# Two banks of 288 columns for each head's scores, and turned tails in the free columns of the PV banks

## The reference, cut to what matters

```python
# q, k, v: (4 batches, 8 heads, 576 tokens, 64)
scores = q @ k.T / 8
thresh = max(scores) - tau
scores = where(scores >= thresh, scores, -1e9)
attn = exp(scores - max(scores)); attn /= sum(attn) + 1e-9
x = attn @ v                        # per head, then (4, 576, 512)
u = x + (relu(x.T @ w_tok1) @ w_tok2).T      # mixing over tokens
y = u + relu(u @ w_ch1) @ w_ch2
h = relu(y @ w_in); z = h * sigmoid(conv3(h)); out = z @ w_out
```

## Time and profile before

| | |
|---|---|
| median of 3 runs | 868.86 us (868.48 to 869.29) |
| profiled execution | 868.8 us, span of the core 867.0 us |
| granted TensorE clock, mean | 0.996 |
| TensorE matmul busy | 826.0 us, 95% of the span, 5512 instructions |
| VectorE, ScalarE, GpSimd busy | 420.9, 411.0, 263.7 us |
| chain that ended last | PE 86%, DVE 5%, ACT 4%, issue 4% |

### The profile page before, as it was taken

The page is one execution under the profiler, slowest core; times in us unless marked ns, Lnnn a source line. Parts: engine busy times, 40 slices in busy tenths (PEclk is TensorE's granted clock), DMA queues, the critical chain, the costliest instruction groups (busy, mean ns, idle before and its releaser), DMA issues.

```text
span 867.0 us, 14725 instructions
## 1 busy us (share of the span) xinstructions
PE 826.0 (95%) x5512; PEld 655.8 (76%) x5512; DVE 420.9 (49%) x829; ACT 411.0 (47%) x866; POOL 263.7 (30%) x202
## 2 busy tenths in 40 slices
PE   7889899999999999799999999999999999999998
PEld 3556566666666666678888888888899989898996
DVE  6787777777777773621121121121122908246280
ACT  4787777777778775311111111121112737356471
POOL 0063323232232321472020020030092645528180
PEclk9999999999999999899999999999999999999999
DMA  9311111111111114000000000000230010010101
GB/s 267 112 50 50 50 51 48 48 48 48 48 48 48 48 17 147 1 1 0 1 1 1 0 1 1 1 0 1 110 85 2 2 50 1 25 36 0 48 0 60
DMA packets 20906, 33.75 MB, mean 39 GB/s; under 512 B 4416, under 2 KB 11136, under 8 KB 20864
## 3 DMA queue, kind: packets, MB, share of 16 engines
q1 hardware_dynamic: 20864, 33.18, 11.8%
HBM read 28.46 MB, written 4.72 MB: 38 GB/s over the span
## 4 chain that ended last, share of the span: by engine, by line
PE 86%; DVE 5%; ACT 4%; issue 4%; DMA 1%; POOL 0%; DVEq 0%; ACTq 0%; SPq 0%; POOLq 0%
PE score L1142 17%; PE score L1253 12%; PE score L987 5%; PE out_t L1157 4%; PE turn_y L1157 4%; PE mixed L1157 4%; PE tails L1157 4%; PE out_t L1053 4%; PE out_t L1238 4%; PE mixed L1053 4%; PE mixed L1099 3%; PE score L1010 3%; PE turn_y L1238 3%; PE mixed L1238 3%; PE tails L1238 3%
## 5 line engine op out<-in xcount | busy, mean ns | idle before, releaser
L903 DVE SCALAR_TENSOR_TENSOR h<-score,h 128x512 fp32r<-128x512 f32 (+1 forms) x60 | 38.3, 638 | 246.6 <-ACT h L683 246.6
L683 ACT ACTIVATE h<-score 128x512 fp32r<-128x512 f32 (+1 forms) x60 | 33.3, 555 | 256.5 <-PE score L1142 256.5
L824 DVE TENSOR_SCALAR_CACHE_REDUCE negs<-score,neg_scale 128x576 f32<-128x576 f32 x144 | 112.6, 815 | 73.5 <-PE score L987 44.8
L841 DVE SCALAR_TENSOR_TENSOR prob<-negs,thresh,exps 128x576 f32<-128x576 f32 x144 | 133.7, 960 | 0.3 <-ACT thresh L595 0.3
L592 ACT ACTIVATE exps<-negs,neg_max 128x576 f32<-128x576 f32 x144 | 104.7, 772 | 2.2 <-DVE negs L824 1.5
L1142 PE MATMUL score<-uh,w1h 128*128 128x512 f32 (+1 forms) x240 | 89.2, 372 | 6.1 <-DVE ul L873 6.1
L1142 PE MATMUL score<-ul,w1h 128*128 128x512 f32 (+1 forms) x240 | 89.0, 371 | 0.0
L1142 PE MATMUL score<-uh,w1l 128*128 128x512 f32 (+1 forms) x240 | 89.0, 371 | 0.0
L560 POOL TENSOR_TENSOR zl<-z,zh 128x512 fp32r<-128x512 f32 x32 | 54.8, 1712 | 98.1 <-ACT zh_t L762 98.1
L1010 PEld LDWEIGHTS score<-ident,prob 64*128 64x128 f32 x512 | 41.0, 139 | 45.3 <-issue 45.2
L987 PE MATMUL score<-qk 64*128 64x512 f32 x256 | 72.3, 641 | 0.0
(11 more groups left out here) (179 smaller groups left out, 2001.0 us busy)
## 6 DMA issues: line engine op xcount, KB each, us to landing
qk<-in_qk SPq DMA_DIRECT2D x16, 704.0 KB, 4.1
vm<-in_v SPq DMA_DIRECT2D x16, 320.0 KB, 4.4
result<-ostage SPq DMA_DIRECT2D x16, 256.0 KB, 2.1
w1f<-in_moe_w_ch SPq DMA_DIRECT2D x4, 768.0 KB, 11.0
w2f<-in_moe_w_ch SPq DMA_DIRECT2D x4, 768.0 KB, 8.1
wif<-in_moe_w_in SPq DMA_DIRECT2D x1, 2048.0 KB, 7.9
wof<-in_moe_w_out SPq DMA_DIRECT2D x8, 256.0 KB, 2.6
wt2f<-in_moe_w_tok SPq DMA_DIRECT2D x1, 576.0 KB, 9.8
```

The source lines that it names most:

```text
L824: nc.vector.tensor_scalar(negs[:, i, h, :], raw_of[h], neg_scale[:, 0:1], None, ALU.mult, ALU.min, accum_out=neg_max[:, i, h:h + 1]).then_ ...
L841: nc.vector.scalar_tensor_tensor(out=prob[:, i, h * S:(h + 1) * S], in0=negs[:, i, h, :], scalar=thresh[:, i, h:h + 1], in1=exps[i][:, h, ...
```

## The change

The scores of a head take two banks, 288 columns in each, with products of 64 rows in four parts (column half c, head h). The product for the tails goes, and with it the doubled k in the input, in which the second head's keys are laid so that its last 64 come first. The waits on `max_done` come one per head. Bank 3 of `score` now belongs to the scores, and the bank once called `tails` (now `turn_x`) takes one half of the turned probabilities. The turned tails go to columns 288 and up of `out_t` and `mixed`: tile 0's in two turns of 64 rows ahead of the PV products, tile 1's behind them, tiles 2 and 3 in s = 2 and 3. ScalarE drains them in four copies where there was one. The output turned back goes to `out_t` in one bank, and the second half of `mix_out(1)`, which is computed in the order mixed, out_t, waits until that is drained.

```diff
-        turn = [score[:, 3, :], turn_y[:, :]]
-        raw = score[:, 0:3, :].rearrange("p b c -> p (b c)")
-        raw_of = [raw[:, 0:S], raw[:, 2 * BANK - TAIL:3 * BANK]]
+        turn = [turn_x[:, :], turn_y[:, :]]
+        raw_of = [score[:, 0:2, 0:HALF], score[:, 2:4, 0:HALF]]
...
-            def drain_tails(at):
-                act.wait_ge(tail_turned, FULL * (at.g + 1))
-                nc.scalar.activation(probTt[at.par][:, 0:MAIN], tails[:, :], ACT.Copy).then_inc(tails_drained, 1)
+            def drain_first_tails(at):
+                if at.k == 0:
+                    act.wait_ge(tail_turned, 2)
+                nc.scalar.activation(probTt[at.par][:, 0:D], mixed[:, TAIL_AT:TAIL_AT + D], ACT.Copy).then_inc(tails_drained, 1)
+                nc.scalar.activation(probTt[at.par][:, D:2 * P], out_t[:, TAIL_AT:TAIL_AT + P + D], ACT.Copy) \
+                    .then_inc(tails_drained, 1)
+            def drain_tail(at, t):
+                act.wait_ge(tail_turned, FULL * at.g + t + 1)
+                bank = out_t if t == 2 else mixed
+                nc.scalar.activation(probTt[at.par][:, t * P:(t + 1) * P], bank[:, TAIL_AT:TAIL_AT + P], ACT.Copy) \
+                    .then_inc(tails_drained, 1)
             def drain_out(pair, k):
                 act.wait_ge(pv_done, pair + 1)
+                if k < PAIRS - 1:
+                    act.wait_ge(tail_turned, FULL * (pair + 1) + 2)
...
-                nc.scalar.activation(uy_pair[:, pair, 0:MAIN], tails[:, :], ACT.Copy).then_inc(xt_drained, 1)
+                nc.scalar.activation(uy_pair[:, pair, 0:MAIN], out_t[:, :], ACT.Copy).then_inc(xt_drained, 1)
...
-            def score_tails(unit):
...
-                    nc.tensor.matmul(raw_tails, qT[par][:, t * P:(t + 1) * P],
-                                     kd[par][:, :].rearrange("p (n c) -> p n c", c=TAIL))
...
+            def scores(unit):
...
+                    for c in range(2):
+                        for h in range(2):
+                            if t >= 1 and c == 0:
+                                pe.wait_ge(max_done, tiles_to(g, t) - 1 + h)
+                            rows = slice(h * D, (h + 1) * D)
+                            mm = nc.tensor.matmul(score[:, 2 * h + c, 0:HALF], qT[par][rows, t * P:(t + 1) * P],
+                                                  kT[par][rows, halves[c]])
                 else:
+                    pe.wait_ge(max_done, tiles_to(g, t) - 1)
+                    for c in range(2):
+                        mm = nc.tensor.matmul(score[:, c, 0:HALF], qd[par][:, :], kT[par][:, halves[c]])
...
+            def turn_first_tails(at):
+                wait_for_banks(at)
+                pe.nop(nofuse=True)
+                for r, bank in enumerate((mixed, out_t)):
+                    rows = slice(r * D, (r + 1) * D)
+                    mm = nc.tensor.transpose(bank[:, TAIL_AT:TAIL_AT + D],
+                                             prob[rows, slot_of(at.k, 0), MAIN:MAIN + 2 * TAIL], ident[rows, rows])
...
             def turn_out(at):
...
+                if at.units:
+                    pe.wait_ge(tails_drained, TAILS * at.g + 3)
...
+            def turn_back(pair):
                 pe.wait_ge(x_done, pair + 1)
-                pe.wait_ge(tails_drained, pair + 2 if k < PAIRS - 1 else PAIRS)
                 for r in range(FULL):
-                    mm = nc.tensor.transpose(tails[:, r * P:(r + 1) * P], x32[:, r, :], ident[:, :])
+                    mm = nc.tensor.transpose(out_t[:, r * P:(r + 1) * P], x32[:, r, :], ident[:, :])
...
             def mix_out(at, i):
...
-                for c, bank in enumerate((out_t, mixed)):
+                for c in (i, 1 - i):
+                    bank = (out_t, mixed)[c]
+                    if at.pv and i == 1 and c == 0:
+                        pe.wait_ge(xt_drained, g)
...
                     if at.units:
                         turn_probs(at, s)
+                        if s == 0:
+                            turn_first_tails(at)
                     if at.pv and s < 2:
-                        times_v(g - 1, k - 1, (2 * s, 2 * s + 1))
-                    if at.units and s < FULL:
-                        turn_tails(at, s)
+                        times_v(at, (2 * s, 2 * s + 1))
                     if at.pv and s == 1:
                         times_v_tail(g - 1, k - 1)
+                    if at.units and s == 1:
+                        turn_tails(at, 1)
```

More of the change, by code:

```diff
@@ L109, in build @@
     sA = Region(w2l_at)
[L110 to L114, removed]
+    qk = [sA.put(f"qk{i}", [P, 2 * S + 2 * TAIL]) for i in range(2)]
+    qT = [x[:, 0:S] for x in qk]
+    kT = [x[:, S:2 * S] for x in qk]
+    qd = [x[:, 2 * S:2 * S + 2 * TAIL] for x in qk]
     negs = sA.put("negs", [P, 2, 2, S])
     exps = [sA.put("exps0", [P, 2, S])]
-    assert sA.at >= w2h_at
+    sA.at = max(sA.at, w2h_at)
     def pair_buffers(region, i):
@@ L655, in drain_x, with drain_u @@
             def drain_x(pair):
-                nc.scalar.activation(uy_pair[:, pair, 0:MAIN], tails[:, :], ACT.Copy).then_inc(xt_drained, 1)
-            def drain_u(pair):
-                for c, bank in enumerate((out_t, mixed)):
-                    act.wait_ge(u_done, 2 * pair + c + 1)
-                    if c == 0 and not (isinstance(pair, int) and pair == 0):
+                nc.scalar.activation(uy_pair[:, pair, 0:MAIN], out_t[:, :], ACT.Copy).then_inc(xt_drained, 1)
+            def drain_u(pair, i):
+                for n in range(2):
+                    c = (n + i) % 2
+                    bank = (out_t, mixed)[c]
+                    act.wait_ge(u_done, 2 * pair + n + 1)
+                    if n == 0 and not (isinstance(pair, int) and pair == 0):
                         act.wait_ge(u_added, pair)
@@ L718, in body @@
                             drain_hidden(at, 1)
+                        if at.units:
+                            drain_tail(at, 3)
                         if PAIRS <= k < PAIRS + 2:
@@ L983, in scores, with turn_short @@
                 par = k % 2
+                halves = [slice(c * HALF, (c + 1) * HALF) for c in range(2)]
+                if t == 0:
+                    pe.wait_ge(qk_loaded[par], LOADS * (g // 2 + 1))
                 if t < FULL:
-                    for h in range(2):
-                        rows = slice(h * D, (h + 1) * D)
-                        mm = nc.tensor.matmul(score[:, 2 * h, :], qT[par][rows, t * P:(t + 1) * P], kT[par][rows, 0:MAIN])
-                else:
-                    mm = nc.tensor.matmul(score[:, 0, :], qd[par][:, :], kT[par][:, 0:MAIN])
+                    if t == 0 and k >= 1:
+                        pe.wait_ge(max_done, tiles_to(g, 0))
+                    for c in range(2):
[5 more added lines that the diff above has]
+                                                  kT[par][rows, halves[c]])
+                else:
+                    pe.wait_ge(max_done, tiles_to(g, t) - 1)
+                    for c in range(2):
+                        mm = nc.tensor.matmul(score[:, c, 0:HALF], qd[par][:, :], kT[par][:, halves[c]])
                 mm.then_inc(s_done, 1)
-            def turn_x_tail():
+            def turn_short():
                 return nc.tensor.transpose(turn[0][:, NT * D:NT * D + TAIL], x32[0:TAIL, FULL, :], ident[0:TAIL, 0:TAIL])
@@ L1033, in turn_tails @@
-                nc.tensor.transpose(tails[:, t * P:(t + 1) * P], prob[:, slot_of(k, t), MAIN:MAIN + 2 * TAIL], ident[:, :]) \
-                    .then_inc(tail_turned, 1)
-            def times_v(pair, k, kts):
+                if t == 1:
+                    to = out_t[:, TAIL_AT + D:TAIL_AT + D + P]
+                elif t == 2:
+                    pe.wait_ge(tails_drained, TAILS * g + 2)
+                    to = out_t[:, TAIL_AT:TAIL_AT + P]
+                else:
+                    if at.pv:
+                        pe.wait_ge(short_x, g)
+                    if at.hid:
+                        pe.wait_ge(hid_left, g - 2)
+                    if at.mix:
+                        pe.wait_ge(u_drained, 2 * (g - 4) + 2)
+                    to = mixed[:, TAIL_AT:TAIL_AT + P]
@@ L1041, in times_v @@
                     pe.wait_ge(turn_drained, 2 * NT * (pair + 1))
[L1042 to L1048, removed]
+                    if not at.units:
+                        wait_for_banks(at)
                 for kt in kts:
@@ L1110, in mix_out @@
                         pe.wait_ge(u_drained, 2 * (g - 4))
+                        pe.wait_ge(xt_drained, PAIRS)
                 else:
                     pe.wait_ge(u_drained, 2 * (g - 3))
-                    if at.pv:
-                        pe.wait_ge(x_done, g)
+                    if at.units:
+                        pe.wait_ge(tails_drained, TAILS * (g + 1))
+                    if at.pv and not at.units:
                         pe.wait_ge(short_x, g)
-                for c, bank in enumerate((out_t, mixed)):
+                for c in (i, 1 - i):
```

(7 more changed lines are left out.)

80 lines of the change are left out of this document (45 added, 35 removed).

## The result

The change makes the kernel 3.4% slower: 898.5 us against 869.1, ratio 1.0335 with a 95% interval of 1.031 to 1.036. I had forecast 866.6 and a range of 860.5 to 872.5. The error is 32 us. Some 22 of them come from two short stretches in a pair of bodies in which TensorE's clock falls to half.

What follows compares the result with a forecast made beforehand. TensorE was taken as nearly full in the attention stage, waiting on VectorE or ScalarE between pairs. Terms -2.1 - 1.8 - 4.8 - 0.45 + 6.6 + 0.3 = -2.25 took 868.8 to 866.6 us; range 860.5 to 872.5.

Steps and rivals of the forecast that it cites:

- rival 3: Idle 2.35 us before mix_out(1)'s second half lowers TensorE's clock: 12 us lost over six bodies, 878.6 us; chance 0.04.
- C: Turn from odd into even body: xl runs before both masks, which end 0.48 earlier; -0.8 each, six bodies, -4.8 us.
- A: Score products: shorter units at s=1 and s=2 gain 0.45 us in every body with PV.
- body 16: Loop body 16: turned-back output goes to the same bank, ScalarE free, wait 0.3; +0.3 us.
- body 15: Loop body 15: no new scores at its end, so it gains only 0.45 us.
- The start: Units before the first PV product: 0.3 each, some seven, less first turns, -2.1 us; first PV product near 28.2.
- bodies 1 and 2: First two bodies with PV: 0.45 from shorter score products and 0.3 twice at their ends; 0.9 each, -1.8 us.
- The score unit: Four half-product steps on TensorE replace main and tail products: 1.06 us for 1.28.
- the cycle of units at the start: First-body cycle: head 0's first half runs under head 1's copy, so 3.30 us becomes 2.98.
- The wait of D: Even into odd body: mix_out(1)'s second half waits 2.35 us for drain_x; loss 1.55, net +1.1 each, six bodies, +6.6.
- The two heads side by side over the wait: Half products of both heads overlap across the new wait; otherwise 10.8 us more, 877.4 us, a rival at chance 0.07.

Runs made afterwards that it cites:

- drain_x_first: Changed kernel with ScalarE's drain of the turned-back output moved ahead of the exponentials of the next pair's tile 1: 872.6 us, ratio 1.0044.
- old_with_wait: Kernel before, own banks and score products, plus only the new order in mix_out(1) and a wait for the drain of x: 882.9 us, ratio 1.0144.
- fill_out_wait: Changed kernel with the first half of mix_out(1) computed three times over, filling the idle time before the out_t wait: 886.1 us, ratio 1.0198.

## Why the prediction was wrong

**The step that failed** is the clock. The sum has no term for it: I had "TensorE's clock at the full value throughout the stage" and left its fall to rival 3 ("The idle 2.35 us lowers TensorE's clock"), at a chance of 0.04 and a price of 12 us. It is 22.5 us (898.5 less 876.0). The last sentence of the prediction looked for the failure in the size of the idle stretch; that was 2.04 us for 2.35 and did not fail. Nearly half of the 22.5 lies in a second place which I did not list: 886.1 less 876.0 = 10.1 us belong to the turn from the odd to the even body (less the one fall at 65 us in that run), where two idle stretches of 0.7 and 1.05 us follow a score unit drawn out to 2.0 us by its waits. I had read one gap of 1.0 us "in slices at the full one" as a clearance for each such gap by itself. In the kernel before the 1.1 us there came 1.8 us behind another stretch of 0.7, with a unit of scores at full density between them; in the changed one that unit is thinned out by the wait inside it. That this is why the clock falls is argued, not shown, and it can't be the whole reason: in `drain_x_first` the same thinned unit and idle stretches of 0.79 and 1.05 us at 173 to 175 us left the clock at 1.00. That it falls there, and what it costs, is shown.

**The term mis-sized besides** is C, -0.8 for each of six odd bodies. At the full clock the odd body is 22.3 us, +0.3: six times 1.1 us. Part C had xl done before both masks, and it stopped there; the next instruction in GpSimd's queue, w1h, was never asked after. With w1h moved the body is 21.5, so w1h makes 0.8 of the 1.1; the rest I put down to xl, which still stands in front of the first mask, without a run that takes it apart. A's share there (shorter score units) only turned into waiting for the mask.

**Waits not seen**: at body 16 the first PV product stands 1.56 us behind the drain of x from `out_t` (page of waits above), since `wait_for_banks` guards the bank that before held only PV sums; it was 0.68 us before. And in body 15 the turn of tile 3's tail into `mixed` waits 0.6 us for ScalarE's work on x (L662). The body from PV start to PV start is 17.64 us at the full clock, forecast 16.52 - 0.45 = 16.07: some 1.6 us.

**The start** gave less: the first PV product is at 29.10, forecast 28.2, before 30.35; bodies 1 and 2 gave 0.65 us each for 0.9. In all 1.4 us; why is open.

Together, 22.5 + 6.6 + 1.6 + 1.4 = 32.1, against 31.9 us between forecast and time.

**What held.** The score unit, 1.07 for 1.06, and the cycle of units at the start, 5.84 to 8.81 = 2.97 us for 2.98. Part A's gain: at the full clock and without the wait the even body is 19.76 (`drain_x_first`), which is 20.22 less 0.46, for 0.45. The wait of D: its place, its cause, its number, 2.04 us for 2.35, and its price at the full clock, 21.28 less 19.76 = 1.52 for 1.55. The two heads side by side over the wait, as the rows had it. The Trainium skill's "TensorE: Matmul & The Clock Gate" (Part 3, what overlaps and what doesn't) says that matmuls start in program order; this trace doesn't agree. Here a turn in rows 0 to 63 starts 0.05 us before the last half product of head 1, which stands ahead of it in the code:

```profile
16.31 0.24 PE L1024 MATMUL turn_x<-ident,prob 64*128 64x64 f32 x1
16.36 0.40 PE L998 MATMUL score<-qk 64*128 64x288 f32 x1
```

## What to carry to other kernels

When an edit adds an idle stretch to a TensorE that was nearly full, price the clock with it: here 29 us of loss were 22.5 of clock and some 7 of waiting (less what the change gains), and the busy share stayed at 95%. Whether the clock falls behind a given stretch of 1 to 2 us could not be foretold from its length here, so it belongs in the range, not in a remote chance. Test it by filling the gap with products that nobody reads; if the kernel gets faster, it is the clock. A bank given a second use needs its drain looked up in the draining engine's order, and where a job on GpSimd moves, the one queued behind it has to be followed as well.

## What was not expected of the hardware

The clock falls after idle stretches shorter than I had taken as harmful: behind 2.04 us in each of six places; behind 2.2 us in four of six in one execution of `old_with_wait`, and by the mean clock in hardly any in its four others; and behind 0.69 and 1.05 us separated by eight turns, 0.46 us. It came back by itself after 3 to 4 us at half behind the wait for `out_t`, and after 3 to 7 us at the other turn.

Where it falls differs from body to body of one run, and from run to run at one place. The kernel after and `fill_out_wait` run the same program up to body 4. Both have idle stretches of 0.4 and 0.7 us at 64 to 65 us, and then, first in the kernel after, second in `fill_out_wait`:

```profile
66.00:68.00 2.00, 2.00 (x18) 0.97 (x16) 2.00 (x7) 2.00 (x4) 1.92 (x3) 1.00 0.00 0
```

```profile
66.00:68.00 2.00, 2.00 (x10) 1.03 (x10) 2.00 (x5) 2.00 (x4) 1.92 (x3) 0.50 0.00 0
```

The times of such kernels spread accordingly: 895.8 to 900.9 us for the kernel after, 868.5 to 869.6 for the one before.
